# Orders of a fused attention and MLP kernel redone, quadrant tiles in rounds, and decayed keys turned by VectorE and 16 transfers

## The reference

```python
for t in range(S):
    cur = np.einsum('bhd,bhe->bhde', u[None] * kt, vt)
    y[:, :, t] = np.einsum('bhd,bhde->bhe', rt, state + cur)
    state = wt[:, :, :, None] * state + np.einsum('bhd,bhe->bhde', kt, vt)
```

## Time and profile before

| | |
|---|---|
| times of three runs | 591.61 (median), 590.94 to 592.5 us |
| the profiled execution | 590.05 us |
| its span, first to last instruction | 588.1 us |
| granted TensorE clock, mean | 0.989 |
| TensorE matmul | 561.5 us busy, 95% |
| VectorE | 316.3 us, 54% |
| ScalarE | 301.1 us, 51% |
| GpSimd | 10.5 us, 2% |
| chain that ended last | TensorE 86%, VectorE 5%, ScalarE 3%, issue 3%, DMA 2% |

### The profile page before, as it was taken

The page is one execution under the profiler, slowest core; times in us unless marked ns, Lnnn a source line. Parts: engine busy times, 40 slices in busy tenths (PEclk is TensorE's granted clock), DMA queues, the critical chain, the costliest instruction groups (busy, mean ns, idle before and its releaser), DMA issues.

```text
span 588.1 us, 15153 instructions
## 1 busy us (share of the span) xinstructions
PE 561.5 (95%) x6279; PEld 513.7 (87%) x6279; DVE 316.3 (54%) x632; ACT 301.1 (51%) x650; POOL 10.5 (2%) x28
## 2 busy tenths in 40 slices
PE   7889989999999999999999999999999999999983
PEld 6788879989979998999999999999999999998332
DVE  8589767747855664456546644565363124323304
ACT  3666635565563456454644564455544456564313
POOL 5010000000000000000000000000000000000000
PEclk9799999999999999999999999999999999999997
DMA  8994623424423332233223322333121297668628
GB/s 283 364 229 158 192 75 98 136 73 117 119 73 86 91 105 67 60 99 97 77 74 101 89 70 76 88 102 85 50 66 28 73 389 230 230 216 288 236 87 321
DMA packets 53733, 80.80 MB, mean 137 GB/s; under 512 B 4304, under 2 KB 33616, under 8 KB 53664
## 3 DMA queue, kind: packets, MB, share of 16 engines
q1 hardware_dynamic: 42160, 54.54, 29.4%
q10 hardware_dynamic: 10704, 22.13, 12.9%
q0 software_dynamic: 800, 3.15, 1.6%
HBM read 70.76 MB, written 9.04 MB: 136 GB/s over the span
## 4 chain that ended last, share of the span: by engine, by line
PE 86%; DVE 5%; ACT 3%; issue 3%; DMA 2%; SPq 0%; DVEq 0%; ACTq 0%
PE hps L1422 33%; PE acc L1557 32%; PE mps L1370 2%; PE zps L1348 2%; PE mps L1456 2%; PE acc L1671 1%; DMA raw<-dmaj 1%; PE mps L1625 1%; DMA out<-obuf 1%; PE mps L1638 1%; PE zps L1354 1%; PE mps L1702 1%; PE mps L1658 1%; PE hps L1702 1%; PE zps L1364 1%
## 5 line engine op out<-in xcount | busy, mean ns | idle before, releaser
L1207 DVE TENSOR_TENSOR gl<-g,gh 128x384 fp32r<-128x384 f32 (+1 forms) x144 | 73.7, 512 | 210.0 <-ACT gh L899 209.8
L1422 PE MATMUL hps<-xh,wi_hi 128*128 128x384 f32 (+1 forms) x432 | 146.4, 339 | 6.0 <-DVE xl L544 4.4
L1422 PE MATMUL hps<-xh,wi_lo 128*128 128x384 f32 (+1 forms) x432 | 137.1, 317 | 0.0
L1422 PE MATMUL hps<-xl,wi_hi 128*128 128x384 f32 (+1 forms) x432 | 136.9, 317 | 0.0
L1557 PE MATMUL acc<-wo_hi,gl 128*128 128x384 f32 x384 | 129.6, 337 | 0.0
L1557 PE MATMUL acc<-wo_hi,gh 128*128 128x384 f32 x384 | 129.2, 336 | 0.3 <-DVE wo_lo L1182 0.3
L1557 PE MATMUL acc<-wo_lo,gh 128*128 128x384 f32 x384 | 129.3, 337 | 0.0
L899 ACT ACTIVATE gh<-g 128x384 fp32r<-128x384 f32 (+1 forms) x144 | 70.5, 490 | 105.2 <-PE acc L1557 104.5
L888 ACT ACTIVATE g<-hps 128x384 f32<-128x384 f32 (+1 forms) x144 | 65.6, 455 | 84.7 <-PE hps L1422 84.3
L1422 PEld LDWEIGHTS hps<-xh,wi_hi 128*128 128x128 f32 x432 | 81.1, 188 | 14.9 <-DVE xl L544 8.6
L1422 PEld LDWEIGHTS hps<-xl,wi_hi 128*128 128x128 f32 x432 | 81.4, 188 | 0.0
(11 more groups left out here) (253 smaller groups left out, 778.9 us busy)
## 6 DMA issues: line engine op xcount, KB each, us to landing
w1s<-w SPq DMA_DIRECT2D x16, 768.0 KB, 6.9
w2s<-w SPq DMA_DIRECT2D x16, 768.0 KB, 6.2
natural<-rknat ACTq DMA_DIRECT2D x21, 384.0 KB, 3.1
vn<-vnat SPq DMA_DIRECT2D x24, 192.0 KB, 2.5
tests<-wall SPq DMA_DIRECT2D x6, 768.0 KB, 13.6
out<-obuf SPq DMA_DIRECT2D x12, 384.0 KB, 3.9
raw<-dmaj ACTq DMA_DIRECT2D x20, 226.2 KB, 2.7
raw<-dmaj ACTq DMA_DIRECT2D x20, 225.8 KB, 2.6
```

What stands on the lines that cost most here:

```text
L1207: dve.tensor_tensor(out=gl[F % 2][:, 0:wide], in0=g32[F % 2][:, 0:wide], in1=gh[F % 2][:, 0:wide].bitcast(fp32), op=ALU.subtract).then_inc ...
L1422: last = pe.matmul(hps[F % 2][:, 0:wide], w[:, g, at:at + 128], v[i % 2][:, g, 0:wide], start=m == 0, stop=m == 3 * G - 1)
```

## The change

- **Keys.** From chunk 10 on (`FLIP`), `turn_keys` and ScalarE's copy are gone. VectorE transposes `kd` (now 128 partitions, the 16 added ones set to zero once for chunks 4 and 5) in blocks of 32x32 into `turned`, and SP puts the 16 block positions in place in `kb` with 16 transfers of 32 partitions by 4 pieces of 128 bytes. State sums of these chunks use 64 key columns instead of 48.
- **Rounds.** In a meeting the four quadrants now get tiles in turn: a crossed sum pair with two straight block products; two crossed block products with two straight state products; two crossed state products with a straight sum pair.
- **Steps.** The meeting (3, none) moves from F=10 to F=11, chunk 2's mask from F=8 to F=7, weight piece 5's low part from F=9 to F=8. From step 3 on, x is split in slots 7, 11, 14 instead of 6, 10, 14. `rest_x` moves ahead of `invert`, `grown_keys` and the rest, `split_x` ahead of the key and output copies, `move_across` to the end of ScalarE's slot.
- **Prologue.** On TensorE `outputs(1)` moves ahead of `permute(0)`; on VectorE `low_part(0)` ahead of `first_output(1)`; on ScalarE `distances(1)` ahead of `turned_keys(1)` and `distances(3)` ahead of `high_first(1)`.

```diff
-        kd = [sb(f"kd{i}", [R, HP, C]) for i in range(2)]
+        kd = [sb(f"kd{i}", [128, HP, C]) for i in range(2)]
...
+        FLIP = BASE[4] + 1
+        first_of_step = [BASE[i + 1] + 1 for i in range(3, NST - 1)]
...
+        def turning(n, on_pe, on_dve):
+            return {"flip": on_dve} if n >= FLIP else {"turn": on_pe}
...
-        place_parts(2, scan=1, invert=1, grow=2, weigh=3, decayed=3, turn=4, mask=8, across=6)
-        place_parts(3, load_n=5, scan=5, invert=6, grow=6, decayed=7, turn=8, weigh=9, across=9)
+        place_parts(2, scan=1, invert=1, grow=2, weigh=3, decayed=3, turn=4, mask=7, across=6)
+        place_parts(3, load_n=5, scan=5, invert=6, grow=6, decayed=7, turn=8, weigh=9, across=10)
...
-        meeting_at = {5: (None, 2), 9: (2, 3), 10: (3, None), 18: (None, 4), 22: (4, 5), 26: (5, 6)}
+        meeting_at = {5: (None, 2), 9: (2, 3), 11: (3, None), 18: (None, 4), 22: (4, 5), 26: (5, 6)}
...
-                        weigh=f - 2, decayed=f - 1, turn=f, across=f + 4)
+                        weigh=f - 2, decayed=f - 1, across=f + 4, **turning(n, f, f - 4))
-                        weigh=f + 4, decayed=f + 5, turn=f + 5, across=f + 8)
+                        weigh=f + 4, decayed=f + 5, across=f + 8, **turning(n + 1, f + 5, f + 3))
-                            weigh=f + 8, decayed=f + 9, turn=f + 9, across=f + 12)
+                            weigh=f + 8, decayed=f + 9, across=f + 12, **turning(n + 2, f + 9, f + 7))
...
+        splits_late = {7: 0, 11: 1, 14: 2}
-        low_at = {0: 2, 4: 3, 9: 5, 10: 6, 12: 7}
+        low_at = {0: 2, 4: 3, 8: 5, 10: 6, 12: 7}
...
+            def spread_keys(n):
+                sp.wait_ge(blocks_turned, n - FLIP + 1)
+                sp.wait_ge(meetings, met_in[n - 2])
+                for j in range(C // BLOCK):
+                    for i in range(FB):
+                        sp.dma_start(kb[n % 2][BLOCK * j:BLOCK * (j + 1), :, i],
+                                     turned[BLOCK * i:BLOCK * (i + 1), j]).then_inc(kb_in[n % 2], 16)
...
                     load_vn(n + 2)
+                late = n + 2 in first_of_step
+                if FLIP <= n + 2 < NCH and not late:
+                    spread_keys(n + 2)
...
                     load_x(n, m, slow)
+                if FLIP <= n + 2 < NCH and late:
+                    spread_keys(n + 2)
...
+            def turn_blocks(n):
+                dve.wait_ge(front, n + 1)
+                if n > FLIP:
+                    dve.wait_ge(kb_in[(n - 1) % 2], 16 * FB * FB * ((n - 1 - FLIP) // 2 + 1))
+                dve.transpose(turned[:, :, :, :].rearrange("t j p d -> t (j p d)"),
+                              kd[n % 2].rearrange("d p (j t) -> d j p t", t=BLOCK)).then_inc(blocks_turned, 1)
...
+                for p in range(HP):
+                    if n is not None:
+                        last = crossed_sums(p)
+                    if p == HP - 1 and n is not None:
+                        last.then_inc(half_summed, 1)
+                    if o is not None:
+                        for c in range(2):
+                            from_block(c, c, p)
+                if o is not None:
                     for p in range(HP):
-                        last = sum_tile(0, 1, p, True)
-                        if both:
-                            last = sum_tile(1, 0, p, True)
-                    last.then_inc(half_summed, 1)
-                if o is not None:
-                    for product in (from_block, from_state):
-                        for p in range(HP):
-                            for c in range(2):
-                                for par in range(2):
-                                    last = product(c, par, p)
+                        for c in range(2):
+                            from_block(c, 1 - c, p)
+                        for c in range(2):
+                            from_state(c, c, p)
                 if n is not None:
                     pe.wait_ge(half_summed, n - PRE + 1)
-                    for p in range(HP):
-                        last = sum_tile(0, 0, p, not both)
-                        if both:
-                            last = sum_tile(1, 1, p, False)
+                for p in range(HP):
+                    if o is not None:
+                        for c in range(2):
+                            last = from_state(c, 1 - c, p)
+                    if n is not None:
+                        last = straight_sums(p)
                 last.then_inc(meetings, 1)
```

More of the change, by code:

```diff
@@ L23 @@
 HALF = 64
+BLOCK = 32
+FB = 128 // BLOCK
 R = HALF + D
@@ L106, in attention_mlp_soft_experts @@
         rp = [sb(f"rp{i}", [R, HP, C]) for i in range(2)]
-        kd = [sb(f"kd{i}", [R, HP, C]) for i in range(2)]
-        kn = [sb(f"kn{i}", [C, HP, R]) for i in range(2)]
+        kd = [sb(f"kd{i}", [128, HP, C]) for i in range(2)]
+        kn_at = [place[0] + i * FB * HP * BLOCK * 4 for i in range(2)]
+        kn = [sb(f"kn{i}", [C, HP, R], at=kn_at[i]) for i in range(2)]
+        kb = [sb(f"kb{i}", [C, HP, FB, BLOCK]) for i in range(2)]
         natural = sb("natural", [C, 2, DM])
@@ L123, in attention_mlp_soft_experts @@
         restart = sb("restart", [R, HP, C + 1])
+        turned = sb("turned", [128, C // BLOCK, HP, BLOCK], at=place[0])
         warm = sb("warm", [128, 640], f32r)
@@ L262, in attention_mlp_soft_experts @@
         kn_done = sem("kn_done")
+        blocks_turned = sem("blocks_turned")
+        kb_in = [sem(f"kb_in{i}") for i in range(2)]
+        pads_zeroed = sem("pads_zeroed")
         z_done = sem("z_done")
@@ L411, in split_now @@
                 return None
-            m = splits[SIZES[i + 1]].get(f) if i else {12: 0, 14: 1}.get(f)
+            m = (splits_late if i >= 3 else splits[SIZES[i + 1]]).get(f) if i else {12: 0, 14: 1}.get(f)
             return None if m is None else (i + 1, m)
@@ L465, in sum_banks @@
                 return zps[0:R, 0:HP * D], yps[0:R, 0:HP * D]
-            return mps[0:R, 0:HP * D], mps[0:R, HP * D:2 * HP * D]
+            return mps[:, 0:HP * D], mps[:, HP * D:2 * HP * D]
         def permuted_x(c):
@@ L863, in start_up @@
                 excesses(0)
+                distances(1)
                 turned_keys(1)
-                distances(1)
                 excesses(1)
@@ L870, in start_up @@
                 high_first(0)
+                distances(3)
                 high_first(1)
-                distances(3)
                 excesses(3)
@@ L931, in _ @@
                     act.dma_start(natural[:, :, :], rknat[n]).then_inc(rows_in, 16)
+                if F is not None and F < NF * NST and split_now(F):
+                    split_x(act, *split_now(F))
                 if (F, "turn") in part_at:
@@ L986, in _ @@
                                        ACT.Copy).then_inc(el_done, 1)
+                if (F, "across") in part_at:
+                    move_across(part_at[F, "across"])
             tail_act(act)
@@ L1057, in grown_keys @@
                 await_field(n, KK)
-                dve.tensor_tensor(out=kd[n % 2][:, :, :], in0=field(n, KK), in1=inv[:, :, 1:C + 1], op=ALU.mult).then_inc(front, 1)
+                if n in (FULL, FULL + 1):
+                    dve.memset(kd[n % 2][96:128, :, :], 0.0).then_inc(pads_zeroed, 1)
+                    dve.wait_ge(pads_zeroed, n - FULL + 1)
+                dve.tensor_tensor(out=kd[n % 2][0:R, :, :], in0=field(n, KK), in1=inv[:, :, 1:C + 1], op=ALU.mult).then_inc(front, 1)
+            def turn_blocks(n):
[4 more added lines that the diff above has]
+                              kd[n % 2].rearrange("d p (j t) -> d j p t", t=BLOCK)).then_inc(blocks_turned, 1)
             def mask_scores(n):
@@ L1083, in first_state @@
             def first_state(n):
-                delta = [ps.rearrange("d (p e) -> d p e", p=HP) for ps in sum_banks(n)]
+                delta = [ps[0:R].rearrange("d (p e) -> d p e", p=HP) for ps in sum_banks(n)]
                 if n < PRE:
@@ L1153, in start_up @@
                 next_state(1)
+                low_part(0)
                 first_output(1)
-                low_part(0)
                 bound_decays(0)
@@ L1210, in _ @@
                     decays(part_at[F, "scan"])
+                if F is not None and F < NF * NST and split_now(F):
+                    rest_x(dve, *split_now(F))
                 if (F, "invert") in part_at:
@@ L1214, in _ @@
                     grown_keys(part_at[F, "grow"])
+                if (F, "flip") in part_at:
+                    turn_blocks(part_at[F, "flip"])
                 if (F, "mask") in part_at:
@@ L1232, in _ @@
                     low_part(low_behind[F])
-                if F is not None and F < NF * NST and split_now(F):
-                    rest_x(dve, *split_now(F))
                 if F == NF * NST + 1:
@@ L1369, in sum_tile, with crossed_sums, straight_sums @@
                     rows = slice(HALF * c, HALF * (c + 1))
```

(31 more changed lines are left out.)

4 lines of the change are left out of this document (removed).

## The result

The changed kernel takes 604.49 us, median of 4 runs (601.64 to 608.57), against 591.72 before: ratio 1.0221, interval 1.0151 to 1.0291. It is slower; 576.1 was forecast, outside the range on the far side. Its profiled execution took 602.48, its span is 600.7.

The account below looks back on a forecast made before the run. TensorE was taken to bound the kernel from 200 to 450 us, with waits before 184. Gains of 1.1 + 3.9 + 2.0 + 5.6 + 2.9 = 15.5 us gave 574.5 profiled, 576.1 median; range 571.5 to 584.

Parts of the forecast that it names:

- part 5: Key transfers on SP: 16 issues per chunk land with 1.5 us margin; late x costs nothing up to gl's need.
- I take 0.45: SP's queue: assumed price in us of one issue of a new key transfer, chosen from rows at 0.42 and once 0.93.
- break-even pace: SP's key issues: at 0.66 us each the gain is used up, 1.7 us per chunk; above that the kernel is slower.
- so no wait: TensorE's need for transferred keys: they land at 198.0 to 198.4, wanted at 199.9, margin 1.5 us.
- Rival (a): SP bounds, keys late: nine chunks each late by 15 x (pace - 0.45) - 1.5; 627 at 0.93; chance 0.15.
- part 2: First steps: hidden layer F=16 starts at 74.6, gain 3.9 us; xl waits at F=32 and F=48 go, 2.0 us.
- Part 1: Prologue: reordering starts the first hidden layer at 32.6 instead of 33.68, gain 1.1 us, bounds 0 and 2.7.
- Rival (d): First steps: early gain absent, the later meeting makes x of chunk 3 late again; 580 us, chance 0.08.
- Part 3: Keys from chunk 10: 14 turnings off TensorE save 5.6 us; VectorE transposes take 0.7 each; 64 columns cost 0, at most 2.
- Part 4: Meetings: new tile order saves 0.20 us each, 0.1 at batch ends; output-only one loses 0.46; net gain 2.9 us.
- (b): Meetings: rounds bring nothing as issue order sets the pace, output-only meetings still lose; 579.5 us, chance 0.10.
- (c): Meetings: two row tiles in one bank run one after the other, 0.54 us longer each, 10.3 us; 586.4, chance 0.04.

Follow-up runs that it names:

- e5: Changed kernel with each chunk's 16 key transfers issued half by SyncE and half by GpSimd, on two queues: 577.59 us, ratio 0.9769 to the kernel before.
- e3: Changed kernel with the same 16 transfers, each writing one 512-byte run per partition (keys in wrong places): 601.12 us, ratio 1.0157 to the kernel before.
- e7: Changed kernel with load_x ahead of the 16 transfer issues for every chunk: 621.97 us, ratio 1.0527 to the kernel before.
- e6: e5 with rest_x back at the end of VectorE's slot in all slots F below 48: 578.85 us, ratio 0.9773 to the kernel before.
- e12: e5 with VectorE's old order (rest_x last) in step 0 only, before slot 16: 576.36 us, ratio 0.9738 to the kernel before.
- e1: Changed kernel with TensorE turning all keys as before, so no block transposes or 16 transfers: 583.0 us, ratio 0.9839 to the kernel before.
- e9: e1 with the old order of meetings, so only the new prologue, slot and x-split orders remain: 588.89 us, ratio 0.9932 to the kernel before.
- e4: Changed kernel with eight transfers of twice the size per chunk (keys in wrong places): 577.94 us, ratio 0.9766 to the kernel before.

## Why the prediction was wrong

**The failed step is in part 5: "I take 0.45".** An issue with its gap measured 0.65 (16 in 10.45 us), over the nine sets 0.67. The text had its break-even pace at 0.66 and the row of 0.93, and took the value of the majority of rows. Those rows were transfers to or from memory outside the core; none had both ends on it, as the new ones have. A row of a different kind bounded the price, and the range should have held it: 0.66 lay between 0.42 and 0.93, so the sign hung on it. With "so no wait" the whole term was put at nothing.

**Rival (a) was the right mechanism, priced too low.** By its formula 0.65 gives 15 x 0.20 - 1.5 = 1.5 us for each of nine chunks, 13.5 in all, 589.6; the mean pace of 0.67 gives 1.8, 16.2 in all, 592.3, the gain used up. Measured are 604.5. From the traces, for the missing 12:

- The nine gaps in TensorE's matmuls are 19.4 us from start to start, of which 0.27 each is the distance before any meeting: 16.9 us lost, 0.7 above the formula. That the formula comes so near is in part luck, for it has no ring in it: in four of the nine a late x delayed the next keys, 3.5 us in all. Part 5 said that a late x "costs nothing" until gl is needed. It had looked at what follows x on TensorE, not at what follows it on VectorE, where this same change had put `rest_x` ahead of invert, grow and turn.
- 2.8 us are in the five slots right behind a late meeting (F=56, 72, 88, 104, 108), which take longer than in e5; TensorE's waits for `grown` are of this kind (2.3 us in four, one of which, 0.56 us at F=19, e5 has too): VectorE makes `grown` behind the same late xl, inverse and turned keys.
- 3.1 us are a gap within the meeting that begins at 277.18, before a straight sum (2.9 in the list of waits, released by nothing that the profile shows). e3, whose keys are late as well, has 2.4 us at the same place; the kernels with keys in time have none, nor has e7, whose keys are later still. Two transfers of instructions (8 and 16 KB) start at 279.65, within the gap, and in e3 at 277.5 and 277.64, where its gap begins. Whether TensorE waited for them isn't shown: the cause stays open.
- About 1.7 us of half clock after the longest wait.
- 3.8 us of early gain, there at F=16 and gone by F=18 (part 2).

Together 0.7 + 2.8 + 3.1 + 1.7 + 3.8 = 12.1.

**Part 1, prologue: not shown.** First layer at 31.95, forecast 32.6. But with the new order twelve profiles have it anywhere from 30.42 to 34.41 (median 31.98), and with the old one two have 33.61 and 35.82; 1.1 can't be told in that.

**Part 2, first steps: right at its slot, wrong in sum.** Hidden layer F=16 came at 74.35 (forecast 74.6), with no wait for xl, and the xl waits at F=32 and F=48 went (without the new order, e6, they are back with 2.0). But 74.6 held no gain of the prologue; with its 1.1 the sum stood for 73.5, and from F=0 to F=16 the gain is 2.55, not 3.9: the wait of 1.6 us for `wo_lo` is new. By F=18 most of the rest is gone, 2.3 for the wait for chunk 4's keys and 1.5 in the slot behind it, at half clock. VectorE bounds that place: it owes TensorE `wo_lo`, xl and the keys, and the order only chooses which comes last. e6 and e12 show the other choice, with no difference in time shown. Part 2 moved `rest_x` and named nothing that stood behind it. Rival (d) had the loss but not its cause, as x of chunk 3 came in time.

**Part 3, keys: right, but 64 columns aren't free.** Fourteen turnings went, and a transpose took 0.71, forecast 0.7:

```profile
L1097 DVE STREAM_TRANSPOSE turned<-kd x14: 702/711/714, 161.3 to 444.3; 128x512 f32<-128x512 f32 x14
```

A full meeting, from the first score to the next layer, fell from 2.19 to 1.88 with 48 key columns and to 1.98 with 64 (e5, four and eleven such meetings, each within 0.01). So 64 cost 0.10 a meeting, 1.1 us in these eleven; 0 had been taken, with 2 as the bound.

**Part 4, rounds: right in kind, larger in size.** Forecast 0.20 a meeting, measured 0.31 at equal columns, and by e1 against e9 5.5 us in all, where 2.9 had been forecast. An output-only meeting took 1.31 instead of 1.05, so +0.26 where 0.46 was forecast. Rivals (b) and (c) are out: by (c) a meeting would take 1.67 - 0.20 + 0.54 = 2.01 us from first sum to next layer, and it took 1.45, as the row shows. So the sum pairs in one bank did not go one after the other. This is against the rule that the prediction took from the Trainium skill, TensorEngine Tiling (Array Packing), section Gotcha 1: PSUM Pressure.

**The sum, with the keys in time, nearly held.** e5 and e12 took 577.59 and 576.36, against 576.1. In profiled executions it is 576.67 and 576.36 against 574.5. In e12 hidden layer F=18 starts 2.0 us earlier than before, where parts 1 and 2 had promised 5.0; from there to F=124 it gains 11.5, where xl waits, keys and rounds had promised 2.0 + 5.6 + 2.9 = 10.5. Too much was promised early and too little late, and that these cancel in part is luck.

## What to carry to other kernels

A transfer between two places on the core cost the queue that issued it about 0.6 us, from 16 to 64 KB alike, so count transfers, not bytes, before scattering blocks: sixteen a chunk were more than 10 us of one engine's time, and as eight on each of two queues they caused no wait. Where work is added to a queue or moved on an engine, list everything behind it up to the next round of the loop, and follow it until the ring closes: here issues delayed x, and x in four of nine cases the next keys. And when break-even lies inside the bounds of a price that no row shows, the chance of the wrong side is that of the price, not of the row most like it.

## What the runs showed of the hardware

- An issue of a transfer with both ends on the core took SyncE 0.59 to 0.64 us, with 128 or 512 pieces, 16 to 64 KB, pieces of 128 bytes or written runs of 512; loads of x took 0.42, stores of y 0.40 each, loads of vn 0.46 (medians). GpSimd took 0.55 for the same transfers. What makes the difference to 0.42 was not tried.
- A wait of 4.24 us was followed by 3.3 us at a granted clock of 0.50; the eight shorter waits for keys, up to 2.3 us from start to start, were not followed by one, nor was the gap of 3.1 us within a meeting. Other runs show it after shorter ones: the clock fell at 394.0 in e3 and at 72.6 in e5, each time behind 1.8 us idle. The gap of 2.56 us before the keys of chunk 4 was followed by one in this kernel; e4 has the same gap and stays at 1.00. The idle 2.4 us before hidden layer F=16 were followed by one in e12, not in e6 and not in the kernel before. So the length of the gap alone does not tell.
